# Opening of a clustered-attention kernel: centroid norms, first pair's operands and arg-max arranged anew

## What is computed

```python
q_n = q / (norm(q) + 1e-6); k_n = k / (norm(k) + 1e-6); c_n = centroids / (norm(centroids) + 1e-6)
q_assign = argmax(q_n @ c_n.T); k_assign = argmax(k_n @ c_n.T)     # one cluster for each token
mask = q_assign[:, None] == k_assign[None, :]
scores = where(mask, (q @ k.T) / 8, -1e9)
out = softmax(scores) @ v
```

## Time and profile before

| | |
|---|---|
| time, median of 3 runs | 716.68 us (716.2 to 717.33) |
| span of the profiled execution | 715.3 us |
| TensorE busy | 679.1 us (95% of the span) |
| VectorE busy | 412.5 us (58%) |
| ScalarE busy | 328.0 us (46%) |
| GpSimd busy | 227.6 us (32%) |
| start of the first score matmul | 24.22 us |

### The profile page before, as it was taken

One profiled execution on the slowest core, in us unless ns is written; L12 is line 12 of the kernel. 1 busy time (PEld: TensorE's weight loads), 2 busy tenths in 40 slices (PEclk: granted clock), 3 DMA queues, 4 the chain that ended last, 5 costly groups with the idle time before them and its releaser, 6 DMA issues.

```text
span 715.3 us, 11565 instructions
## 1 busy us (share of the span) xinstructions
PE 679.1 (95%) x4153; PEld 642.8 (90%) x4153; DVE 412.5 (58%) x682; ACT 328.0 (46%) x638; POOL 227.6 (32%) x166
## 2 busy tenths in 40 slices
PE   3699999999999999899999999999998899999998
PEld 3598898989898988789999999999997899999998
DVE  2488979898988988445212303412389834783133
ACT  1578778787879787524401201302455504421010
POOL 7419462525345384401500000100175502361000
PEclk9999999999999999999999999999999899999999
DMA  6555536354453351010300000000321100000022
GB/s 199 133 133 156 134 80 156 78 148 96 102 132 66 88 154 45 6 39 7 128 14 1 1 1 0 21 23 1 100 77 45 60 0 2 1 1 1 0 81 97
DMA packets 16608, 46.62 MB, mean 65 GB/s; under 512 B 2752, under 2 KB 4800, under 8 KB 16576
## 3 DMA queue, kind: packets, MB, share of 16 engines
q1 hardware_dynamic: 16576, 46.18, 23.9%
HBM read 24.15 MB, written 3.15 MB: 38 GB/s over the span
## 4 chain that ended last, share of the span: by engine, by line
PE 84%; DVE 10%; issue 2%; ACT 2%; SPq 0%; DMA 0%; DVEq 0%; POOL 0%; POOLq 0%; ACTq 0%
PE ps L442 17%; PE ps L444 17%; PE ps L443 17%; PE ps L479 7%; PE ps L487 5%; PE ps L471 4%; PE ps L488 4%; PE ps L472 4%; PE ps L452 3%; PE ps L463 2%; DVE pt_lo L996 1%; PE ps L494 1%; DVE turn L1105 1%; DVE z_s L1110 1%; DVE turn L1103 1%
## 5 line engine op out<-in xcount | busy, mean ns | idle before, releaser
L968 DVE TENSOR_REDUCE neg_max<-ps 128x1 f32<-128x768 f32 x96 | 91.6, 954 | 26.3 <-PE ps L472 23.9
L996 DVE TENSOR_TENSOR pt_lo<-ps,pt_hi 128x384 fp32r<-128x384 f32 x192 | 97.5, 549 | 12.0 <-ACT pt_hi L735 11.1
L735 ACT ACTIVATE pt_hi<-ps 128x384 fp32r<-128x384 f32 x192 | 84.5, 489 | 37.5 <-PE ps L479 36.1
L755 ACT ACTIVATE prob<-ps,neg_max 128x768 f32<-128x768 f32 x96 | 86.9, 905 | 13.9 <-DVE neg_max L968 12.6
L839 ACT ACTIVATE g_s<-ps 128x384 fp32r<-128x384 f32 x48 | 23.6, 492 | 139.1 <-PE ps L444 139.1
L444 PE MATMUL ps<-u_s,ch_s 128*128 128x384 f32 (+1 forms) x256 | 85.5, 334 | 0.0
L442 PE MATMUL ps<-u_s,ch_s 128*128 128x384 f32 (+1 forms) x256 | 85.5, 334 | 0.0
L443 PE MATMUL ps<-u_s,ch_s 128*128 128x384 f32 (+1 forms) x256 | 85.5, 334 | 0.0
L479 PE MATMUL ps<-ident,prob 128*128 128x128 f32 x576 | 82.4, 278 | 1.4 <-DVE pt_lo L996 1.3
L479 PEld LDWEIGHTS ps<-ident,prob 128*128 128x128 f32 x576 | 67.2, 143 | 10.1 <-DVE pt_lo L996 2.9
L487 PE MATMUL ps<-pt_lo,v_s 128*128 128x384 f32 x192 | 70.2, 366 | 4.8 <-DVE o_sum L975 4.8
(11 more groups left out here) (130 smaller groups left out, 1507.6 us busy)
## 6 DMA issues: line engine op xcount, KB each, us to landing
stage<-ch_dram SPq DMA_DIRECT2D x9, 768.0 KB, 4.3
qa<-pair_s SPq DMA_DIRECT2D x32, 192.0 KB, 3.0
ka<-pair_s SPq DMA_DIRECT2D x32, 192.0 KB, 3.9
raw<-q_dram SPq DMA_DIRECT2D x8, 384.0 KB, 4.3
raw<-k_dram SPq DMA_DIRECT2D x8, 384.0 KB, 4.4
raw_v<-v_dram SPq DMA_DIRECT2D x8, 384.0 KB, 4.2
qb<-pair_s SPq DMA_DIRECT2D x16, 192.0 KB, 3.4
kb<-pair_s SPq DMA_DIRECT2D x16, 192.0 KB, 4.1
```

Of the source, the lines that this page charges most:

```text
L735: return act.activation(o, i, ACT.Copy)
L755: act.activation(prob[:, slot, :].rearrange("p (c k) -> p c k", c=2), ps[:, 2 * slot:2 * slot + 2, 0:HS], ACT.Exp, bias=neg_max[:, s:s + 1 ...
L968: dve.tensor_reduce(neg_max[:, s:s + 1], ps[:, 2 * slot2:2 * slot2 + 2, 0:HS], AX.XY, ALU.max, negate=True).then_inc(s_max, 1)
L996: dve.tensor_tensor(pt_lo[at], ps[:, 4 + u, 0:HS].rearrange("p (k q) -> p k q", k=HT), pt_hi[at], ALU.subtract).then_inc(s_pt_lo, 1)
```

## The change

The centroids come first, in one DMA that the host has laid out transposed (128 x 64: partitions 64 j to 64 j + 63 are the values of head j of each pair, columns 4 x 16). Their norms come from one matmul of the squares with `same_head` (a block matrix of ones and zeros), which gives every partition its column's sum; VectorE scales all 64 columns at once, straight into `cen_t`, which it has cleared before.

Pair 0's q and k get a buffer of their own, `raw0`, so that `load_qk(1)` no longer waits for the sims. ScalarE scales q of pair 0 (before, GpSimd did) and writes the hi parts of head 0 into `qa`, `ka` (twice) and `qb`; VectorE writes its two lo parts. `stack(0, 0)` falls away. GpSimd's split of pair 0 remains for head 1, and starts behind `s_k0_lo`, VectorE's last operand write. The arg-max of pair 0 works on 12 x 16 similarities at a time (`argmax_first`), queries and then keys, each on a PSUM bank of its own.

```diff
-            load_qk(0)
-            sp.wait_ge(s_const, 1)
-            for h in range(H):
-
-                c0 = (h % 2) * D
-                sp.dma_start(cen[h * C:(h + 1) * C, c0:c0 + D], cent[h]).then_inc(s_cen, 16)
+            sp.dma_start(cen[:].rearrange("p h c -> p (h c)"), cent).then_inc(s_cen, 16)
+            sp.dma_start(raw0[:, 0, :], q[0]).then_inc(s_raw_q0, 16)
+            sp.dma_start(raw0[:, 1, :], k[0]).then_inc(s_raw_k0, 16)
+            load_qk(1)
             load_v(0)
             load_weights(0)
             load_weights(1)
-            stack(0, 0)
-            sp.wait_ge(s_sims, 1)
-            load_qk(1)
             stack(0, 1)
...
+            def split_first():
+
+                rounded(pair_s[:, 1, 0, :], raw0[:, 1, :], [P, S]).then_inc(s_qk_split, 1)
+                pool.wait_ge(s_q0_scaled, 1)
+                rounded(pair_s[:, 0, 0, :], raw0[:, 0, :], [P, S]).then_inc(s_qk_split, 1)
+                pool.wait_ge(s_qk_split, 2)
+                for i in range(2):
+                    pool.tensor_tensor(pair_s[:, i, 1, :], raw0[:, i, :], pair_s[:, i, 0, :],
+                                       ALU.subtract).then_inc(s_qk_split, 1)
...
-            scale_q(0)
-            split_qk(0, first=True)
+            pool.wait_ge(s_k0_lo, 1)
+            split_first()
+            scale_q(1)
             split_v(0, 0, first=True)
             split_v(0, 1, first=True)
-            scale_q(1)
             pair(0, first=True, weights=(*W_TOK1, *W_TOK2))
...
-            pe.wait_ge(s_const, 8)
-            pe.wait_ge(s_cen_n, 1)
-            pe.transpose(ps[:, 0, 0:P], cen_n[:], ident[:]).then_inc(s_cen_pe, 1)
-            pe.wait_ge(s_cen_t, 2)
-            sims(0, 0)
-            sims(0, 1)
-            pe.wait_ge(s_onehot, 1)
-            oh_transpose(0, 0)
-            pe.wait_ge(s_qoh, 1)
-            oh_transpose(0, 1)
+            pe.wait_ge(s_same_head, 4)
+            pe.wait_ge(s_cen_dve, 1)
+            pe.matmul(ps[:, 0, 0:H // 2 * C], same_head[:], cs[:, 0, :], start=True, stop=True).then_inc(s_cen_pe, 1)
+            pe.wait_ge(s_cen_t, 4)
+            pe.wait_ge(s_q0_scaled, 1)
+            sims(0, 0, src=raw0, first=True)
+            pe.wait_ge(s_raw_k0, 16)
+            sims(0, 1, src=raw0, bank=4, first=True)
+            pe.wait_ge(s_const, 7)
+            for side in range(2):
+                pe.wait_ge(s_onehot, side + 1)
+                oh_transpose(0, side, bank=6 - side)
...
-            act.wait_ge(s_cen_dve, 2)
-            act.activation(cs[:, 1:2], cs[:, 0:1], ACT.Sqrt).then_inc(s_cen_sqrt, 1)
             act.wait_ge(s_cen_pe, 1)
-            for b in range(B):
-                copy(cen_t[:, b, :], ps[:, 0, 0:P]).then_inc(s_cen_t, 1)
-
-            def query_rows(h, j):
+            act.activation(cs[:, 1, :], ps[:, 0, 0:H // 2 * C], ACT.Sqrt).then_inc(s_cen_sqrt, 1)
+            act.wait_ge(s_raw_q0, 16)
+            act.activation(raw0[:, 0, :], raw0[:, 0, :], ACT.Copy, scale=SCALE).then_inc(s_q0_scaled, 1)
+            act.wait_ge(s_q0_scaled, 1)
+            copy(qa[0:D, 0, :], raw0[0:D, 0, :]).then_inc(s_q0_hi, 1)
+            act.wait_ge(s_raw_k0, 16)
+            copy(ka[0:D, 0, :], raw0[0:D, 1, :]).then_inc(s_k0_hi, 1)
+            copy(ka[D:P, 0, :], raw0[0:D, 1, :]).then_inc(s_k0_hi, 1)
+            copy(qb[0:D, 0, :], raw0[0:D, 0, :]).then_inc(s_q0_hi, 1)
...
+            dve.wait_ge(s_cen, 16)
+            flat = cen[:].rearrange("p h c -> p (h c)")
+            dve.tensor_tensor(cs[:, 0, :], flat, flat, ALU.mult).then_inc(s_cen_dve, 1)
+            square = ps[:, 0, 0:H // 2 * C]
             dve.wait_ge(s_cen_sqrt, 1)
-            dve.tensor_scalar(small(2), small(1), 1e-30, None, ALU.max).then_inc(s_cen_dve, 1)
+            dve.tensor_scalar(cs[:, 2, :], cs[:, 1, :], 1e-30, None, ALU.max).then_inc(s_cen_dve, 1)
...
+            dve.wait_ge(s_q0_hi, 1)
+            dve.tensor_tensor(qa[D:P, 0, :], raw0[0:D, 0, :], qa[0:D, 0, :], ALU.subtract).then_inc(s_q0_lo, 1)
+            dve.wait_ge(s_k0_hi, 1)
+            dve.tensor_tensor(kb[0:D, 0, :], raw0[0:D, 1, :], ka[0:D, 0, :], ALU.subtract).then_inc(s_k0_lo, 1)
...
+            def argmax_first(side):
+
+                r = slice(12 * side, 12 * side + 12)
+                sim = ps[:, 4 if side else 7, 0:24 * C].rearrange("p (n c) -> p n c", c=C)
+                shape = [P, 12, C]
+                dve.wait_ge(s_sims, side + 1)
+                dve.tensor_reduce(am1[:, r], sim[:, r, :], AX.X, ALU.max).then_inc(s_am0, 1)
...
-            for step in range(5):
-                argmax(0, step)
+            for side in range(2):
+                argmax_first(side)
```

More of the change, by code:

```diff
@@ L96, in clustered_mixer @@
                 x_t = sb(a2, "x_t", [P, 2, DT, HS], F32)
+        with ExitStack() as r0:
+            raw0 = sb(r0, "raw0", [P, 2, S], F32, side="right")
         with ExitStack() as r:
@@ L376, in pair @@
                 if not last:
-                    split_qk(p + 1)
+                    split_qk(p + 1, second=first)
                 if not first:
@@ L503, in next_score @@
                     q_of = p + n12 // 12
-                    pe.wait_ge(s_stack[j], 96 * q_of + 96)
+                    if first_of_all:
+                        pe.wait_ge(s_q0_hi, 2)
+                        pe.wait_ge(s_k0_hi, 2)
+                        pe.wait_ge(s_q0_lo, 1)
+                        pe.wait_ge(s_k0_lo, 1)
+                    else:
+                        pe.wait_ge(s_stack[j], 96 * q_of + 96 * j)
                     pe.wait_ge(s_qoh, h + 1)
@@ L789, in pair @@
                         mask_rows(2 * p + 2, 0)
[L791 to L792 removed]
+            query_rows(0, 0, bank=6)
+            mask_rows(0, 0, bank=5)
             exp(0, 0, 0)
@@ L920, in _ @@
         def _(dve):
-            def small(i, n=P):
-                return cs[0:n, i:i + 1]
-            dve.wait_ge(s_cen, 16 * H)
+            for j in range(2):
+                for i in range(2):
+                    dve.memset(same_head[j * D:(j + 1) * D, i * D:(i + 1) * D], float(i == j)).then_inc(s_same_head, 1)
             for c in range(C):
                 dve.memset(order[:, c:c + 1], float(C - c))
-            dve.tensor_tensor(cen_n[:], cen[:], cen[:], ALU.mult).then_inc(s_cen_dve, 1)
@@ new lines, in _ @@
+            for b in range(B):
+                for j in range(2):
+                    r = slice(j * D, (j + 1) * D)
+                    dve.tensor_tensor(cen_t[r, b, :].rearrange("p (h j c) -> p h j c", j=2, c=C)[:, :, j, :], cen[r, :, :],
+                                      cs[r, 6, :].rearrange("p (h c) -> p h c", c=C), ALU.mult).then_inc(s_cen_t, 1)
+            dve.wait_ge(s_q0_hi, 1)
+            dve.tensor_tensor(qa[D:P, 0, :], raw0[0:D, 0, :], qa[0:D, 0, :], ALU.subtract).then_inc(s_q0_lo, 1)
@@ new lines, in _ @@
+            dve.wait_ge(s_k0_hi, 1)
+            dve.tensor_tensor(kb[0:D, 0, :], raw0[0:D, 1, :], ka[0:D, 0, :], ALU.subtract).then_inc(s_k0_lo, 1)
+            sim = ps[:, 7, 0:24 * C].rearrange("p (n c) -> p n c", c=C)
+            hot = onehot[:].rearrange("p s t j c -> p (s t j) c")
+            def argmax_first(side):
[4 more added lines that the diff above has]
+                dve.tensor_reduce(am1[:, r], sim[:, r, :], AX.X, ALU.max).then_inc(s_am0, 1)
+                dve.wait_ge(s_am0, 4 * side + 1)
+                dve.tensor_tensor(cand[:, r, :], sim[:, r, :], am1[:, r].unsqueeze(2).broadcast_to(shape),
+                                  ALU.is_ge).then_inc(s_am0, 1)
+                dve.wait_ge(s_am0, 4 * side + 2)
+                dve.tensor_tensor(cand[:, r, :], cand[:, r, :], order[:].unsqueeze(1).broadcast_to(shape),
+                                  ALU.mult).then_inc(s_am0, 1)
+                dve.wait_ge(s_am0, 4 * side + 3)
+                dve.tensor_reduce(am2[:, r], cand[:, r, :], AX.X, ALU.max).then_inc(s_am0, 1)
+                dve.wait_ge(s_am0, 4 * side + 4)
+                dve.tensor_tensor(hot[:, r, :], cand[:, r, :], am2[:, r].unsqueeze(2).broadcast_to(shape),
+                                  ALU.is_equal).then_inc(s_onehot, 1)
```

91 lines of the change are left out of this document (50 added, 41 removed).

## The result

| | before | after |
|---|---|---|
| median | 716.54 us (4 runs, 716.2 to 717.33) | 712.64 us (4 runs, 712.06 to 712.79) |
| ratio, 95% interval | | 0.9942 [0.9928, 0.9955] |
| span of the profiled execution | 715.3 us | 710.7 us |
| first score matmul starts | 24.22 us | 19.34 us |

The changed kernel is faster by 0.58%: 3.9 us by these medians, against 5.4 forecast. The measured 712.64 lies in the range of 708.2 to 714.3. The two profiled spans differ by 4.6 us. In later comparisons the kernel before had medians of 716.96 (9 runs), 716.88 (25) and 717.38 (8), so 3.9 is the low side of what the medians give; the difference from 716.96 is 4.3.

The account below looks back on a forecast made before the run. TensorE was taken to bound the kernel once scores run, behind an opening chain on TensorE, VectorE and ScalarE. First score 24.22 - 18.8 = 5.4 us earlier, so 716.68 - 5.4 = 711.3 us; range 708.2 to 714.3.

Parts of the forecast that it names:

- A first score that starts earlier ends the kernel earlier: Whole kernel: TensorE's time bounds it once scores run, so a first score x us earlier ends it x us earlier.
- the rival of a smaller gain: TensorE's slow pace lasts longer from its first score, one more stretch costing 1.7 us: 713.7 or so; chance 0.15.
- Centroid load and norms: Opening chain: centroids land at 2.6 us, squares start 2.65, reciprocals take 0.55 each, `cen_t` is written by 6.9.
- q and k: Pair 0's loads land at 4.2 and 5.4 us; ScalarE's copies take 0.80 each, done long before they are wanted.
- The rival in which the first loads share the engines with later ones: Slower: q and k land at about 12.8 us with loads issued behind them, score 25.5, 718 us; chance 0.05.
- The new neighbour: Pair 0's arg-max: VectorE instructions with two SBUF operands wait for GpSimd's running one; score at 18.2 or 19.45, middle 18.8.
- Case B: The queries' `cand` times `order` misses GpSimd's boundary at 10.35 and ends at 12.0; keys' `onehot` 17.6, score 19.45.
- the third step for the queries: `cand` times `order`, third of five arg-max steps, two SBUF operands; meets GpSimd's boundary at 10.35, ending 10.7 or 12.0.
- the rival without blocking: Arg-max half-steps fall between GpSimd's instructions, or GpSimd starts later: score 16.05, 8.2 us earlier, 708.5; chance 0.20.
- A: The queries' `cand` times `order` slips in at GpSimd's boundary and ends at 10.7; keys' `onehot` 16.35, score 18.2.
- Behind the first score: After the first score: stack(0, 1), `v` and GpSimd's split of pair 1 come in time; costed at nothing, cover 11.8 us.
- The sum: Whole kernel: first score from 24.22 to 18.8 us, so 5.4 us off; span 709.9, median 711.3.

Follow-up runs that it names:

- e4: Changed kernel with the centroid load issued behind q and k of pair 0 instead of ahead of them; median 715.17 us.
- e1: Changed kernel with GpSimd's opening list held until both arg-max halves end, one wait changed; median 709.91 us, ratio to before 0.9898.
- e6: Changed kernel without direct operand writes for head 0: GpSimd scales and splits pair 0 at once, stacks go through DMA; median 716.24 us, ratio 0.9987.
- e8: The kernel before, unchanged, profiled once more for its spread; median 717.22 us, span 714.8 us.
- e9: Changed kernel with VectorE's addition of 1e-9 to the sums of exponentials left out, the reciprocal reading `den` itself; median 709.89 us, ratio 0.9893.
- e11: Kernel before with only VectorE's addition of 1e-9 to the sums of exponentials left out; median 714.57 us, ratio 0.9958.

## Why the prediction was right, and where it was off

**A first score that starts earlier ends the kernel earlier.** Right in kind. The lead of 4.89 at the first row maximum was 4.6 in the span. It stayed between 4.88 and 4.93 up to the 26th row maximum, so TensorE's slow stretch at its first scores wasn't longer than before: the rival of a smaller gain didn't come true.

**Centroid load and norms.** The squares came at 2.59 (forecast 2.65), the reciprocals of 64 columns took 0.55 as worked out from 6 ns a column, and the sims started at 7.10 (forecast 6.9). e4 confirmed that this chain decides. The estimate of 0.69 us for a reciprocal, which the prediction worked out from the Trainium skill's page "VectorE: DVE Perf Modes" (section "First, the fixed hardware budget"), isn't borne out by the trace: 0.55.

**q and k.** ScalarE's copies took 0.84 instead of 0.80, k landed at 5.7 instead of 5.4; both hidden, as costed. The rival in which the first loads share the engines with later ones is refuted by the landings of 3.0 and 4.0 us.

**The new neighbour.** Right, and it is the step on which the sum rested. Case B came: the third step for the queries didn't slip in at the boundary (GpSimd's second rounding had started at 10.52, the step at 10.69). The four contended steps ended at 12.19, 14.07, 15.95 and 17.49, forecast 12.0, 13.95, 15.95 and 17.6, and the score of that case was forecast at 19.45, measured 19.34. e1 proves the cause and prices it at 3.06 us; the rival without blocking forecast a score at 16.05, and e1 measured 16.28. The Trainium skill's page "SBUF — State Buffer" (section "SBUF: two separate sides") has this as a lock held for a whole instruction, and the trace agrees: 0.36 us became 1.50. The error was to take the middle of A and B, 18.8: 0.54 us of the 5.4. The rule that the prediction drew, that one operand doesn't wait, was read too widely. The `cen_n` line of 1.52 us in the kernel before, the scale of 64 columns in e6 (1.36 instead of 0.20) and `rden` in e1 (2.56 instead of 0.16) are each a `tensor_scalar`: one SBUF tensor and a constant, or a scalar for each partition. They waited; reductions and reciprocals didn't. It did no harm to the sum, because no `tensor_scalar` lies beside GpSimd's list in the changed opening.

**Behind the first score.** Costed at nothing. No wait for a stack or `v` appeared, but 0.5 us went in the loop, at VectorE's jump. It is the second mis-sized term, and nothing in the prediction looked at it.

**The sum.** 24.22 - 19.34 = 4.88 at the score, less 0.5 in the loop, is 4.4 at the last row maximum, and 4.6 in the span. The rest to 3.9 lies in the runs: single executions of the kernel before had spans from 714.2 to 716.7 in the later comparisons. An execution's time was 1.8 us over its span, not 1.4; the 1.4 came of comparing one profile with the median of others. By that distance the profiled execution of the kernel before took about 717.1 us, 0.5 more than the median, and that of the changed kernel took 712.50, 0.1 less. That is the 0.7 between 4.6 and 3.9. So part of the distance to the forecast 5.4 is the spread of single executions: e8 started its first score 0.33 us later than the first profile of the same kernel and had a span 0.5 us shorter.

## What to carry to other kernels

When work is moved between engines, ask what GpSimd is doing while VectorE runs its instructions with two SBUF operands, or SBUF-to-SBUF with a scalar: a step of 0.36 us here cost up to 1.5 us, one of 0.16 us up to 2.56. Moving GpSimd's list out of one chain can put it into the next: here it left the norms and met the arg-max, which took back 3.1 us. Hold GpSimd's list back behind a short latency-bound chain on VectorE (e1: one wait, 3 us at the first score, 2.2 at the end of attention), and look for small VectorE instructions of these kinds beside GpSimd's long ones (e9, e11: 2 to 3 us, most of them at a single place). Cutting a chain's steps in two pays only when nothing stands between the halves (1.8 us without contention, -0.4 with it), and a small load on which the start hangs belongs ahead of large ones on its queue. A loss that grows with the passes of a loop is found by noting at which instruction of each pass the lead steps down.

## What the runs showed of the hardware that I had not expected

- A VectorE instruction of 3 columns with a scalar constant waited 2.4 us for a GpSimd instruction on 1536 columns (e1: 2.56 us for `rden<-den`, 0.16 undisturbed), while a reciprocal of the same columns didn't wait (0.17). A `tensor_scalar` of one column, at 8.56 us in the kernel before, took 0.15 beside GpSimd's second rounding (7.79 to 9.30).
- Between four VectorE writes queued in a row, GpSimd's instructions took their turn after every one: 5.90 us instead of 0.97 for the four (e6).
- A load of 32 KB issued behind two of 384 KB took 4.0 us to be there, against 1.8 as the first of its queue (e4 and the changed kernel).
- A reciprocal on VectorE costs about 6 ns a column beyond a fixed 0.16 us: 164 ns on one column, 0.55 us on 64.
- VectorE's jump back to the start of a loop left it idle for 0.19 to 0.23 us in the kernel before and 0.32 to 0.36 in the changed one, whose loop does the same work. No idle time stood there in the kernels without the addition and its wait (e9, e11).
